# A linear-attention, gated and routed kernel: the first loads in another order, and the product of w3 and w_out one step sooner

## The chip, the cores and the metric

The kernel runs on one core of one Trainium2 chip. The metric is the device time of one execution in microseconds. Before the change three executions took 2084.07, 2080.27 and 2076.05 us, a median of 2080.27 us.

## What is computed

Three stages follow each other, all in float32.

```
for t in range(S):                      # S = 768, for 4 batches x 8 heads of size 48
    y[t] = r[t] @ (state + outer(u * k[t], v[t]))
    state = w[t][:, None] * state + outer(k[t], v[t])
x  = y as (3072, 384)
x2 = ((x @ w1) * (x @ w2)) @ w3 @ w_out        # w1, w2: 384 x 1024; w3: 1024 x 1024; w_out: 1024 x 384
P  = exp(x2 @ w_gate - max), then 8 rounds of row and column normalising
out = sum over 8 experts e of P[:, e] * (relu(x2 @ W1[e]) @ W2[e])
```

The kernel multiplies w3 by w_out once, at its start, into W (1024 x 384), and uses W for every token.

## The kernel before, in words

The tokens of the first stage are cut into 12 units of 256 tokens (`U`). A loop over steps s, which every engine goes through in its own program, does eight steps per unit (`NF = 8`): for s = 8u + k, TensorE makes the small products of unit u (k = 0: `diag`; k = 1 to 7: `score(u, k - 1)`, one level of a tree that combines decayed blocks), and between them other work. After each `score`, VectorE scales R and K by the decays (`level`, L1105), ScalarE copies R into Rpad (`pad`, L814), and only then can the next `score` run. For u = 1 and later TensorE also closes the unit before (`turn_keys`, `update`, `make_y`).

Beside this, in the first fifteen steps, the weights are prepared. TensorE turns w3 in 16 half rows (`turn_w3`, L1384; two turns for each of the eight 512 KB blocks that `load_w3` fetches into four buffers, `RAW = 4`); ScalarE copies each turned half to SBUF (`copy_w3T`, L859); TensorE makes 64 small products with w_out (`make_W`, L1395), five in a step (`W_EACH = 5`), each seen as two matmul records of 128x384. ScalarE and VectorE split each finished block of W into a high and a low part (`copy_W`, `split_W`), and, in steps 9 to 14, split the six parts of w1 and w2 (`copy_wab`, L869; `split_wab`, L1160). Which turn and which products fall into which step is set by `turns_in` and `W_steps` (L398, L399) from `W_FROM = 3`: turns from step 2 on, products from step 3 to 15.

The second stage follows the first by `LAG = 16`: the first `go_up` (x times w1 and w2) stands in step 15 behind `score(1, 6)` and that step's `make_W`, and waits until all six parts of w1 and w2 are split (`wab_split`, L1501). The first `go_down` (times W) is in step 16 and waits for all of W. From then on each step has one `go_up` and one `go_down`. The routed stage, the longest, comes after the twelve units.

The loads of this stage are issued by SyncE (SP), in program order on one queue: K and R of unit 0 (after VectorE or GpSimd has cleared the tiles: `k_set`, `r_set`), `left`, then, when the decays `Wt` of unit 0 have landed, w3's first block and w_out (L456 to L458). Then K and R of unit 1, w3's second block, Wt of unit 1 and so on, each behind a `scored` or `w3_turned` count (L459 to L486). ScalarE's queue carries u, the constants and Wt of unit 0 (L899 to L905). GpSimd's queue loads the experts' weights, the first 576 KB at 37.5 us. TensorE waits for the constants before anything else, and for w_out before the first `make_W` (L1398), and it works strictly in program order: what stands behind a waiting product waits too.

Of the kernel before, what the change touches and what calls it, by code (L numbers as in the profile page):

```python
# [9 lines left out]
def build_program(nc, consts, left, rT, kT, wT, v, uT, moe_w1, moe_w2, moe_w3, moe_w_out, w_gate, w12, out):  # L10
# [10 lines left out]
    B, H, HD, S = rT.shape  # L21
# [9 lines left out]
    HROW = 64  # L31
# [10 lines left out]

    LAG = 16
    W_FROM = 3
    SLICES = NF * U
    RAW = 4
    TURNED = 4
# [43 lines left out]
    with ExitStack() as ctx:  # L92
# [4 lines left out]
        def sb(name, shape, dt=f32, at=None):  # L97
            if at is None:
                at = top[0]
                top[0] += size_of(shape)  # L100
            return nc.alloc_sbuf_tensor_at(name, shape, dt, offset=at)

        def sem(name):
            return ctx.enter_context(nc.semaphore(name))
# [18 lines left out]
        const_sb = sb("const_sb", [P, P + SUB + 2])  # L123
        ident = const_sb[:, 0:P]
        ident32 = const_sb[:, P:P + SUB]
        usel_sb = sb("usel_sb", [P, 2, PAIRS])
# [16 lines left out]
        R = [sb(f"R{p}", [P, PAIRS * CT]) for p in range(2)]  # L143
# [31 lines left out]
        def end_of(limit):  # L175
# [71 lines left out]
        k_loaded, r_loaded, v_loaded = ([sem(f"{n}_loaded{p}") for p in range(2)] for n in ("k", "r", "v"))  # L247
        wab_loaded = [sem(f"wab_loaded{m}") for m in range(2)]
        w3_loaded = [sem(f"w3_loaded{i}") for i in range(RAW)]
        w_loaded, u_loaded, consts_loaded, left_loaded, wout_loaded, wg_loaded, first_loaded, p_stored = map(  # L250
            sem, ["w_loaded", "u_loaded", "consts_loaded", "left_loaded", "wout_loaded", "wg_loaded", "first_loaded", "p_stored"])
        p_loaded = [sem(f"p_loaded{i}") for i in range(2)]
        w2_loaded = [sem(f"w2_loaded{i}") for i in range(2)]
        k_set, k1_set, r_set, rp_set, rp_first, rp_begun, warm_set, w_set, u_set, cleared, w3_turned, w3T_copied = map(
            sem, ["k_set", "k1_set", "r_set", "rp_set", "rp_first", "rp_begun", "warm_set", "w_set", "u_set", "cleared", "w3_turned", "w3T_copied"])
        W_made, W_hi_made, W_split, wab_hi_made, wab_split = map(
            sem, ["W_made", "W_hi_made", "W_split", "wab_hi_made", "wab_split"])
        ruk_made, diag_made, near_set, near_done, scored, r_scaled, k_scaled, decayed, rp_copied = map(
            sem, ["ruk_made", "diag_made", "near_set", "near_done", "scored", "r_scaled", "k_scaled", "decayed", "rp_copied"])
# [24 lines left out]
        PAIR_LOAD = 16 * 2  # L284
        pair_no = lambda u: u // 2 + 1
        level_no = lambda u, l: NL * u + l + 1
# [62 lines left out]
        def last_projection(n):  # L349

            v, o = divmod(n, 6)
            st, _, end = SPANS[v]
            f = NF * end - 1
            G = group_of(st, f)
            return 3 * (block_no(G) + 2 * (f - first_f(G))) + o
# [41 lines left out]

        turns_in = lambda s: [i for i in range(2 * NF) if W_FROM - 1 + HB * i // W_EACH == s]  # L398
        W_steps = lambda s: range(W_EACH * max(0, s - W_FROM), max(0, min(W_EACH * (s + 1 - W_FROM), NF * NF)))  # L399
        W_in = lambda s: [f for f in range(NF) if NF * f + NF - 1 in W_steps(s)]  # L400
# [9 lines left out]
        def part(src, u, h):  # L410
            b, n = divmod(u, UB)
            return src[b, h::2, :, CT * n:CT * n + CT].rearrange("g d t -> d g t")

        rows_of = lambda t, h: by_pair(t[HROW * h:HROW * h + HD, :])
# [3 lines left out]
        def _(sp):  # L418
            def load_k(u):
                for h in range(2):  # L420
                    sp.dma_start(rows_of(K[u % 2], h), part(kT, u, h)).then_inc(k_loaded[u % 2], 16)

            def load_r(u):
                for h in range(2):
                    sp.dma_start(rows_of(R[u % 2], h), part(rT, u, h)).then_inc(r_loaded[u % 2], 16)
# [5 lines left out]
            def load_v(u):  # L431
                b, n = divmod(u, UB)
                sp.dma_start(V[u % 2][:, :, :], v[b, CT * n:CT * n + CT, :].rearrange("(c p) d -> p c d", p=P)).then_inc(v_loaded[u % 2], 16)

            def load_w3(f):
                sp.dma_start(w3_raw[f % RAW][:, :], moe_w3[P * f:P * f + P, :]).then_inc(w3_loaded[f % RAW], 16)

            def load_wab(i, w):
                own = w[0:2 * LAST * HD, :].rearrange("(t h e) f -> h e t f", h=2, e=HD)
                gap = w[2 * LAST * HD:D, :].rearrange("(h t q) f -> h q t f", h=2, q=GAP)  # L440
                for h in range(2):
                    sp.dma_start(wab_raw[HROW * h:HROW * h + HD, i, :, :], own[h]).then_inc(wab_loaded[i], 16)
                    sp.dma_start(wab_raw[HROW * h + HD:HROW * h + HROW, i, :, :], gap[h]).then_inc(wab_loaded[i], 16)
# [6 lines left out]

            sp.wait_ge(k_set, 1)
            load_k(0)
            sp.wait_ge(r_set, 1)
            load_r(0)
            sp.dma_start(left_sb[:, :, :], left).then_inc(left_loaded, 16)
            sp.wait_ge(w_loaded, PAIR_LOAD)  # L456
            load_w3(0)
            sp.dma_start(wout_raw[:, :, :], moe_w_out.rearrange("(j p) d -> p j d", p=P)).then_inc(wout_loaded, 16)  # L458
            sp.wait_ge(scored, level_no(0, 0))  # L459
            sp.wait_ge(k1_set, 1)  # L460
            load_k(1)
            sp.wait_ge(r_set, 2)
            load_r(1)
            load_w3(1)
            sp.wait_ge(decayed, level_no(0, 0))
            sp.wait_ge(scored, level_no(0, 1))
            load_w(1)
# [2 lines left out]
            load_v(0)  # L470
            sp.wait_ge(scored, level_no(0, 3))
            load_w3(3)
            sp.wait_ge(scored, level_no(0, 4))
            load_wab(0, moe_w1)
            sp.wait_ge(scored, level_no(0, 5))
            sp.wait_ge(w3_turned, 2)
            load_w3(RAW)
            sp.wait_ge(scored, level_no(0, 6))
            sp.wait_ge(w3_turned, 4)
            load_w3(RAW + 1)  # L480
            load_v(1)
            sp.wait_ge(w3_turned, 6)
            load_w3(RAW + 2)
            load_wab(1, moe_w2)
            sp.wait_ge(w3_turned, 8)
            load_w3(RAW + 3)  # L486
            assert NF == RAW + 4

            for u in range(1, U + 1):
# [320 lines left out]
        def _(act):  # L810
            def copy(dst, src):
                return nc.scalar.activation(dst, src, ACT.Copy)  # L812
# [83 lines left out]

            act.wait_ge(warm_set, 1)
            copy(warm[:, 1:2], warm[:, 0:1])
            act.wait_ge(u_set, 1)  # L899
            for h in range(2):  # L900
                act.dma_start(usel_sb[HROW * h:HROW * h + HD, h, :], uT[h]).then_inc(u_loaded, 16)
            act.dma_start(const_sb[:, :], consts).then_inc(consts_loaded, 16)
            act.wait_ge(w_set, 1)
            for h in range(2):
                act.dma_start(rows_of(Wt, h), part(wT, 0, h)).then_inc(w_loaded, 16)  # L905
# [172 lines left out]
        def _(dve):  # L1078
            ve = nc.vector
# [92 lines left out]

            ve.memset(warm[:, 0:1], 0.0).then_inc(warm_set, 1)
            ve.memset(K[0][:, :], 0.0).then_inc(k_set, 1)
            ve.memset(Wt[:, :], 0.0).then_inc(w_set, 1)
            ve.memset(usel_sb[:, :, :], 0.0).then_inc(u_set, 1)

            def split_xs(st, p):
                what = x_tile(st, X_OWN[p]) if p in X_OWN else xw[:, :] if p == S3 else xs_sum[:, p, :]
# [568 lines left out]
```

## Time and profile before

| what | value |
|---|---|
| median of three executions | 2080.27 us |
| the profiled execution, its own time | 2073.27 us |
| its span in the trace | 2071.4 us |
| TensorE busy | 2012.6 us, 97% |
| VectorE, ScalarE, GpSimd busy | 66%, 38%, 30% |
| mean DMA traffic | 153 GB/s |

All times below are microseconds from the start of the span. A line of the timeline has start, duration, engine, source line, operation, the tiles written and read, shape, and in brackets how long the engine had been idle and what it waited for. SPq and ACTq lines are issues of DMAs. Matmul ends are modelled.

### The profile page before, as it was taken

What the parts mean: (1) busy time and instruction counts of PE and PEld (TensorE: products, weight loads), DVE (VectorE), ACT (ScalarE), POOL (GpSimd) and SP (SyncE); (2) the same over time, 40 slices, a digit from 0 to 9 for tenths busy, and PEclk for the clock granted to TensorE, in tenths of its full rate; (3) what the DMA queues carried; (4) which work ended last, traced back from release to release, by engine and by line L of the source; (5) the groups of instructions that cost most, each with busy time, mean ns of one, the idle gap of its engine ahead of it and who ended that gap; (6) DMA issues with size and microseconds to landing.
All of it is one profiled execution on the core that took longest, in us unless ns stands there. A gap on an engine that the chain in (4) does not pass through costs nothing.

```text
span 2071.4 us, 40274 instructions
## 1 busy us (share of the span) xinstructions
PE 2012.6 (97%) x16048; PEld 1672.6 (81%) x16048; DVE 1357.8 (66%) x2129; ACT 790.9 (38%) x1448; POOL 614.1 (30%) x879
## 2 busy tenths in 40 slices
PE   6899999999999999999989999999999999999999
PEld 4699999999777777787868888888877888888887
DVE  3677777783686777777676556655676665566556
ACT  4555554553433333333433333332333333333332
POOL 2466776760565666762030000000020000000000
PEclk9999999999999999999999999999999999999999
DMA  8443343330366676775433444343443445443442
GB/s 214 108 122 98 114 130 99 109 104 18 101 229 224 222 248 241 250 256 200 170 122 132 171 146 161 122 167 136 155 140 113 150 140 175 138 160 132 152 137 97
DMA packets 118585, 316.11 MB, mean 153 GB/s; under 512 B 11920, under 2 KB 45616, under 8 KB 118400
## 3 DMA queue, kind: packets, MB, share of 16 engines
q1 hardware_dynamic: 102768, 259.38, 38.7%
q0 software_dynamic: 14944, 53.68, 7.5%
q8 instruction: 128, 2.10, 0.4%
q10 hardware_dynamic: 688, 0.48, 0.1%
q14 instruction: 57, 0.47, 0.1%
HBM read 239.87 MB, written 71.27 MB: 150 GB/s over the span
## 4 chain that ended last, share of the span: by engine, by line
PE 84%; DVE 8%; issue 3%; ACT 2%; DMA 1%; SPq 0%; POOL 0%; DVEq 0%; ACTq 0%
PE ps L1576 22%; PE ps L1578 22%; PE ps L1577 21%; PE ps L1380 4%; PE ps L1381 3%; PE ps L1382 3%; PE ps L1453 2%; PE ps L1403 2%; DVE tb L1306 1%; DVE xs_lo L1082 1%; PE ps L1492 1%; PE ps L1494 1%; DVE tb L1269 1%; DVE R L1117 1%; ACT h_hi L1009 1%
## 5 line engine op out<-in xcount | busy, mean ns | idle before, releaser
L1009 ACT ACTIVATE h_hi<-tb 128x512 fp32r<-128x512 f32 x378 | 239.0, 632 | 651.4 <-DVE tb L1306 619.8
L1576 PE MATMUL ps<-h_hi,w 128*128 128x512 f32 x1152 | 454.7, 395 | 4.2 <-DVE h_lo L1274 4.0
L1578 PE MATMUL ps<-h_hi,w 128*128 128x512 f32 x1152 | 455.3, 395 | 0.0
L1577 PE MATMUL ps<-h_lo,w 128*128 128x512 f32 x1152 | 454.0, 394 | 0.0
L812 ACT ACTIVATE tb<-ps 128x512 f32<-128x512 f32 x378 | 224.8, 595 | 332.2 <-PE ps L1578 325.9
L1274 DVE SCALAR_TENSOR_TENSOR h_lo<-tb,h_hi 128x512 fp32r<-128x512 f32 x382 | 281.3, 736 | 98.6 <-ACT h_hi L1009 79.6
L1265 DVE TENSOR_TENSOR tb<-tb,ps 128x512 f32<-128x512 f32 x252 | 172.1, 683 | 227.7 <-PE ps L1578 227.3
L1269 DVE TENSOR_TENSOR tb<-ps,tb 128x512 f32<-128x512 f32 x252 | 172.8, 686 | 148.1 <-PE ps L1578 148.1
L1306 DVE SCALAR_TENSOR_TENSOR tb<-tb,Pb 128x512 f32<-128x512 f32 x348 | 253.8, 729 | 18.1
L1576 PEld LDWEIGHTS ps<-h_hi,w 128*128 128x128 f32 x1152 | 216.2, 188 | 57.6 <-issue 7.6
L1577 PEld LDWEIGHTS ps<-h_lo,w 128*128 128x128 f32 x1152 | 217.3, 189 | 50.6
L1578 PEld LDWEIGHTS ps<-h_hi,w 128*128 128x128 f32 x1152 | 216.2, 188 | 49.5
L1576 PE MATMUL ps<-xs_hi,early 128*128 128x512 f32 x504 | 201.3, 399 | 5.7 <-DVE tb L1265 3.0
L738 POOL TENSOR_TENSOR xs_sum<-x 128x512 f32<-128x512 f32 x21 | 34.6, 1660 | 559.3 <-PE ps L1578 559.1
L1578 PE MATMUL ps<-xs_hi,early 128*128 128x512 f32 x504 | 200.0, 397 | 0.0
L1577 PE MATMUL ps<-xs_lo,early 128*128 128x512 f32 x504 | 198.4, 394 | 0.0
L1576 PE MATMUL ps<-xs_hi,late 128*128 128x512 f32 x441 | 174.5, 396 | 8.8 <-DVE tb L1269 5.8
L1578 PE MATMUL ps<-xs_hi,late 128*128 128x512 f32 x441 | 173.2, 393 | 0.0
L1577 PE MATMUL ps<-xs_lo,late 128*128 128x512 f32 x441 | 172.8, 392 | 0.0
L812 ACT ACTIVATE Rpad<-R 64x512 f32<-64x512 f32 (+1 forms) x170 | 110.6, 650 | 162.4 <-DVE R L1117 155.1
L1380 PE MATMUL ps<-x,wab_hi 128*128 128x256 f32 x576 | 171.0, 297 | 1.0 <-DMA x<-yT 1.0
L1382 PE MATMUL ps<-x,wab_lo 128*128 128x256 f32 x576 | 161.8, 281 | 0.0
(159 smaller groups left out, 3299.7 us busy)
## 6 DMA issues: line engine op xcount, KB each, us to landing
early<-w_rows SPq DMA_DIRECT2D x63, 1024.0 KB, 5.5
late<-w_rows SPq DMA_DIRECT2D x63, 896.0 KB, 5.2
w<-w_rows SPq DMA_DIRECT2D x128, 384.0 KB, 4.3
w_rows<-batch POOLq DMA_DIRECT2D x105, 384.0 KB, 3.6
w_rows<-w SPq DMA_DIRECT2D x64, 384.0 KB, 2.7
Pb<-p_rows SPq DMA_DIRECT2D x24, 512.0 KB, 6.0
w_raw<-w POOLq DMA_DIRECT2D x16, 576.0 KB, 6.0
w_raw<-w SPq DMA_DIRECT2D x16, 576.0 KB, 4.7
```

What stands on the lines that cost most here:

```text
L812: return nc.scalar.activation(dst, src, ACT.Copy)
L1009: nc.scalar.activation(h_hi[:, slot_of(G, b), :], tb[:, t_of(G, b), :], ACT.Relu).then_inc(h_hi_made, 1)
L1265: ve.tensor_tensor(t, t, bank, ALU.subtract).then_inc(added, 1)
L1269: ve.tensor_tensor(t, bank, t, ALU.add).then_inc(added, 1)
L1274: ve.scalar_tensor_tensor(out=h_lo[:, slot, :], in0=what, scalar=0.0, in1=h_hi[:, slot, :].bitcast(f32), op0=ALU.max, op1=ALU.subtract).th ...
L1306: ve.scalar_tensor_tensor(out=t, in0=what, scalar=0.0, in1=Pb[k % 2][:, 1 - b % 2, :], op0=ALU.max, op1=ALU.mult).then_inc(scaled, 1)
L1380: mm(o, w_hi, x_hi, start=start, stop=False, skip_group_check=shared)
L1381: mm(o, w_hi, x_lo, start=False, stop=False, skip_group_check=shared)
L1382: return mm(o, w_lo, x_hi, start=False, stop=stop, skip_group_check=shared)
L1576: mm(o, w_hi, x_hi, start=start, stop=False, skip_group_check=True)
L1577: mm(o, w_hi, x_lo, start=False, stop=False, skip_group_check=True)
L1578: return mm(o, w_lo, x_hi, start=False, stop=stop, skip_group_check=True)
```

## The change

SP first loads K, then u, the constants and `left`, and, waiting for nothing more, w3's first block and w_out. R of unit 0 moves to ScalarE's queue, ahead of Wt; VectorE clears `usel_sb` before `Wt`. w3's second block goes ahead of K and R of unit 1. The gates' weights (`load_wab`) move behind w3's fifth and sixth blocks (the w1 half) and behind its last (the w2 half), and the waits for `scored(0, 4)` and `scored(0, 6)` go. `W_FROM = 2` moves every turn of w3 and every product of W one step sooner: turns in steps 1 to 13, products in steps 2 to 14.

```
-    W_FROM = 3
+    W_FROM = 2
@@ SP
             load_k(0)
-            sp.wait_ge(r_set, 1)
-            load_r(0)
+            sp.wait_ge(u_set, 1)
+            for h in range(2):
+                sp.dma_start(usel_sb[HROW * h:HROW * h + HD, h, :], uT[h]).then_inc(u_loaded, 16)
+            sp.dma_start(const_sb[:, :], consts).then_inc(consts_loaded, 16)
             sp.dma_start(left_sb[:, :, :], left).then_inc(left_loaded, 16)
-            sp.wait_ge(w_loaded, PAIR_LOAD)
             load_w3(0)
             sp.dma_start(wout_raw[:, :, :], moe_w_out.rearrange("(j p) d -> p j d", p=P)).then_inc(wout_loaded, 16)
             sp.wait_ge(scored, level_no(0, 0))
+            load_w3(1)
             sp.wait_ge(k1_set, 1)
             load_k(1)
             sp.wait_ge(r_set, 2)
             load_r(1)
-            load_w3(1)
...
             load_w3(3)
-            sp.wait_ge(scored, level_no(0, 4))
-            load_wab(0, moe_w1)
             sp.wait_ge(scored, level_no(0, 5))
             sp.wait_ge(w3_turned, 2)
             load_w3(RAW)
-            sp.wait_ge(scored, level_no(0, 6))
             sp.wait_ge(w3_turned, 4)
             load_w3(RAW + 1)
+            load_wab(0, moe_w1)
             load_v(1)
             sp.wait_ge(w3_turned, 6)
             load_w3(RAW + 2)
-            load_wab(1, moe_w2)
             sp.wait_ge(w3_turned, 8)
             load_w3(RAW + 3)
+            load_wab(1, moe_w2)
@@ ScalarE
-            act.wait_ge(u_set, 1)
+            act.wait_ge(r_set, 1)
             for h in range(2):
-                act.dma_start(usel_sb[HROW * h:HROW * h + HD, h, :], uT[h]).then_inc(u_loaded, 16)
-            act.dma_start(const_sb[:, :], consts).then_inc(consts_loaded, 16)
+                act.dma_start(rows_of(R[0], h), part(rT, 0, h)).then_inc(r_loaded[0], 16)
             act.wait_ge(w_set, 1)
@@ VectorE
             ve.memset(K[0][:, :], 0.0).then_inc(k_set, 1)
+            ve.memset(usel_sb[:, :, :], 0.0).then_inc(u_set, 1)
             ve.memset(Wt[:, :], 0.0).then_inc(w_set, 1)
-            ve.memset(usel_sb[:, :, :], 0.0).then_inc(u_set, 1)
```

## Rows read from the trace of the kernel before

**Rows 1.** The page: engines' busy time, and shares of the chain that ended last.
```profile
PE 2012.6 (97%) x16048; PEld 1672.6 (81%) x16048; DVE 1357.8 (66%) x2129; ACT 790.9 (38%) x1448; POOL 614.1 (30%) x879
...
PE 84%; DVE 8%; issue 3%; ACT 2%; DMA 1%; SPq 0%; POOL 0%; DVEq 0%; ACTq 0%
```

**Rows 2.** Stretches: PE, PEld, DVE, ACT, POOL busy; granted clock; DMA share; GB/s.
```profile
0.00:26.44 26.44, 9.59 (x274) 7.20 (x274) 11.03 (x20) 8.63 (x12) 10.24 (x12) 1.00 0.87 204
26.44:62.44 36.00, 36.00 (x578) 24.48 (x579) 16.45 (x31) 20.02 (x36) 4.22 (x6) 1.00 0.94 202
62.44:64.86 2.42, 0.00 (x0) 0.00 (x0) 1.00 (x1) 1.36 (x2) 0.00 (x0) 1.00 1.07 237
64.86:92.00 27.14, 24.27 (x357) 16.57 (x356) 19.16 (x29) 14.99 (x24) 11.87 (x13) 1.00 0.27 68
...
98.00:640.00 542.00, 530.46 (x8667) 486.75 (x8666) 387.74 (x681) 263.99 (x547) 331.41 (x496) 1.00 0.39 117
```

**Rows 3.** Timeline of TensorE and VectorE from 8 to 28 us.
```profile
8.50 1.29 DVE L1094 TENSOR_TENSOR ruk<-K,R 128x512 f32<-128x512 f32 x2 [5.46 <-DMA R<-rT]
...
10.77 1.08 PE L1453 MATMUL ps<-Rpad,K 128*32 128x32 f32 x64
...
14.14 1.09 PE L1453 MATMUL ps<-Rpad,K 128*32 128x32 f32 x64 [2.29 <-ACT Rpad L812]
15.24 1.97 PE L1392 MATMUL ps<-const_sb,w_raw 128*128 128x128 f32 x8
...
17.48 1.08 PE L1453 MATMUL ps<-Rpad,K 128*32 128x32 f32 x64 [0.28 <-issue]
...
20.34 3.49 PE L1403 MATMUL ps<-wout_raw,w3T 128*128 128x384 f32 x10 [1.77 <-DMA wout_raw<-moe_w_out]
...
26.44 0.66 PE L1392 MATMUL ps<-const_sb,w_raw 128*128 128x128 f32 x4 [2.61 <-DMA w_raw<-moe_w]
...
27.03 0.77 PE L1453 MATMUL ps<-Rpad,K 128*32 128x32 f32 x64
...
40.16 1.04 PE L1392 MATMUL ps<-const_sb,w_raw 128*128 128x128 f32 x8
```

**Rows 4.** DMA issues at 3.4, 4.9, 11.3, 27.8 and 52.8 us: KB, us to landing.
```profile
R<-rT SPq DMA_DIRECT2D x1, 192.0 KB, 5.0
...
Wt<-wT ACTq DMA_DIRECT2D x1, 192.0 KB, 6.0
...
wout_raw<-moe_w_out SPq DMA_DIRECT2D x1, 1536.0 KB, 9.0
...
w_raw<-moe_w SPq DMA_DIRECT2D x1, 512.0 KB, 4.0
...
R<-rT SPq DMA_DIRECT2D x2, 192.0 KB, 15.2
```

**Rows 5.** Stretches by DMA traffic, columns as in Rows 2.
```profile
11.90:18.20 6.30, 3.77 (x125) 3.30 (x129) 4.63 (x8) 3.49 (x6) 0.00 (x0) 1.00 1.02 350
...
33.30:53.20 19.90, 19.90 (x278) 13.42 (x277) 7.08 (x15) 11.14 (x22) 3.75 (x5) 1.00 1.03 235
```

**Rows 6.** Timeline of 72 to 92 us: the end of the preparation of the weights.
```profile
72.13 0.68 DVE L1094 TENSOR_TENSOR ruk<-K,R 128x512 f32<-128x512 f32 x1
...
76.58 0.60 ACT L812 ACTIVATE w3T<-ps 128x512 f32<-128x512 f32 x1 [0.51 <-PE ps L1392]
...
87.21 1.27 ACT L812 ACTIVATE Rpad<-R 64x512 f32<-64x512 f32 x2 [3.22 <-DVE R L1117]
...
88.50 0.49 ACT L812 ACTIVATE W_hi<-ps 128x384 fp32r<-128x384 f32 x1
...
89.60 2.85 PE L1403 MATMUL ps<-wout_raw,w3T 128*128 128x384 f32 x8
...
90.59 1.25 DVE L1082 TENSOR_TENSOR wab_lo<-wab_raw,wab_hi 128x1024 fp32r<-128x1024 f32 x1 [1.01 <-ACT wab_hi L812]
...
91.99 0.57 PE L1380 MATMUL ps<-x,wab_hi 128*128 128x256 f32 x1
```

More of the change, by code:

```diff
@@ L44, in build_program @@
     LAG = 16
-    W_FROM = 3
+    W_FROM = 2
     SLICES = NF * U
@@ L452, in _ @@
             load_k(0)
-            sp.wait_ge(r_set, 1)
-            load_r(0)
+            sp.wait_ge(u_set, 1)
+            for h in range(2):
+                sp.dma_start(usel_sb[HROW * h:HROW * h + HD, h, :], uT[h]).then_inc(u_loaded, 16)
+            sp.dma_start(const_sb[:, :], consts).then_inc(consts_loaded, 16)
             sp.dma_start(left_sb[:, :, :], left).then_inc(left_loaded, 16)
-            sp.wait_ge(w_loaded, PAIR_LOAD)
             load_w3(0)
@@ L459, in _ @@
             sp.wait_ge(scored, level_no(0, 0))
+            load_w3(1)
             sp.wait_ge(k1_set, 1)
@@ L463, in _ @@
             load_r(1)
-            load_w3(1)
             sp.wait_ge(decayed, level_no(0, 0))
@@ L472, in _ @@
             load_w3(3)
-            sp.wait_ge(scored, level_no(0, 4))
-            load_wab(0, moe_w1)
             sp.wait_ge(scored, level_no(0, 5))
@@ L477, in _ @@
             load_w3(RAW)
-            sp.wait_ge(scored, level_no(0, 6))
             sp.wait_ge(w3_turned, 4)
             load_w3(RAW + 1)
+            load_wab(0, moe_w1)
             load_v(1)
@@ L483, in _ @@
             load_w3(RAW + 2)
-            load_wab(1, moe_w2)
             sp.wait_ge(w3_turned, 8)
             load_w3(RAW + 3)
+            load_wab(1, moe_w2)
             assert NF == RAW + 4
@@ L898, in _ @@
             copy(warm[:, 1:2], warm[:, 0:1])
-            act.wait_ge(u_set, 1)
+            act.wait_ge(r_set, 1)
             for h in range(2):
-                act.dma_start(usel_sb[HROW * h:HROW * h + HD, h, :], uT[h]).then_inc(u_loaded, 16)
-            act.dma_start(const_sb[:, :], consts).then_inc(consts_loaded, 16)
+                act.dma_start(rows_of(R[0], h), part(rT, 0, h)).then_inc(r_loaded[0], 16)
             act.wait_ge(w_set, 1)
@@ L1174, in _ @@
             ve.memset(K[0][:, :], 0.0).then_inc(k_set, 1)
+            ve.memset(usel_sb[:, :, :], 0.0).then_inc(u_set, 1)
             ve.memset(Wt[:, :], 0.0).then_inc(w_set, 1)
-            ve.memset(usel_sb[:, :, :], 0.0).then_inc(u_set, 1)
             def split_xs(st, p):
```

## The prediction

> **What bounds the kernel now.** I read the page first. TensorE is busy 97% of the span and carries 84% of the chain that ended last [rows 1], so an edit counts only by how much sooner TensorE gets through its program. The stretches say where it is not full: 9.59 of the first 26.44 us, everything from there to 62.44, nothing in 2.42 us at 62.44, 24.27 of 27.14 up to 92.00, then 530.46 of 542 [rows 2]. The change touches only what lies ahead of 92 us; behind that TensorE runs with 98% busy on the same instructions, so a shift of the first `go_up` (91.99) passes to the end one for one. The timeline of the head [rows 3] gives its waits: ruk from 8.50 (R landed), the second score at 14.14, the first `make_W` at 20.34 (w_out landed), the second turn at 26.44 (w3's second block landed).
>
> The whole head idle is 16.85 us, and of what the edits can reach (26.44 - 8.50) only a few us can go. 0.5% of the time, about what a measurement of this kernel can tell from no change, is 10.4 us. That settles most of the chances.
>
> **R on ScalarE's queue, constants behind K.** Before, K and R stand on one queue, u, constants and Wt on the other. R's second half is issued at 3.38 and lands 5.0 later, at 8.4; the last of Wt, from 4.9, + 6.0 = 10.9 [rows 4]. All of it is 1152 + 121 = 1273 KB in the 7 us from the first data (about 3.9) to 10.9: 182 GB/s, and the bytes are the same after the change. What changes is the order. K and R, 768 KB, now come first with nothing between: 768 / 182 = 4.2 us, so 8.1 at this rate; since K was already moving before R's first issue, and some 0.15 MB of the other queue no longer goes ahead, I take 7.5. Constants and `left` follow at about 8.5 to 9.3 (they landed at 9.1 before), so ruk runs at 7.5 to 8.8 and the first score about 1 us sooner, from 9.8 instead of 10.77. Bounds: 0 to 1.2 us sooner.
>
> **Wt behind R, beside w3.** Wt shares the DMA engines with constants and then with w3, whose rows are 4 KB against 1 KB. Alone it would land at 10.5; with w3's 512 KB ahead of it entirely, 512 / 350 = 1.5 us later [rows 5], 12.0. I take 11.5. The first decay scaling began at 11.91, so the head gains 0.4 there (from +0.1 to -1.1), and the second score moves to about 13.8. Little hangs on it: behind it comes the wait for w_out [rows 3].
>
> The Trainium skill (DMA: Bandwidth & Descriptors, "Issuing engines are not separate DMA queues") states that transfers started by different engines interleave on the same 16 DMA engines, and that a second issuing engine saves only issue time. The two queues' 182 GB/s together agree. By that rule alone R would gain 0.7 us (its earlier issue), by mine 0.9, and neither reaches TensorE's end.
>
> **w3's first block and w_out.** This is the term that counts. They were issued at 10.91 and 11.30; data moved from 11.90 to about 18.2 at 350 GB/s [rows 5], and w_out landed at 11.3 + 9.0 = 20.3 [rows 4]: 6.3 us of transfer and 2.1 of tail. Now they stand behind the rest with no pause: the engines are through with the first 1273 KB at about 10.6 instead of idling to 11.9. So w_out lands at 10.6 + 6.3 + 2.1 = 19.0, 1.3 us sooner, though it is issued 6 us sooner: the transfer, not the issue, was the limit. Bounds: 17.0 (the first loads mix with the long rows and nothing of the tail stays) to 20.3.
>
> **One step sooner.** Turns 0 and 1 now stand behind the first score. w3's block lands at 12.5 to 13, the turns take 1.97 [rows 3] and end by 15, which can push the second score to 15; it is still ahead of w_out. But the third score, which ran at 17.48 while TensorE waited for w_out, now stands behind the first `make_W` and waits with it. From w_out's landing to the score of step 4 TensorE now has: five products 3.42 (steady advance; the row shows 3.49), turn 0.53, score 0.69, five products 3.42, turn 0.45, some 8.5 in all, so the score of step 4 begins at 19.0 + 8.5 = 27.5; before it began at 27.03. TensorE is thus 0.5 later by the step, and one block of products ahead. w3's second block, now directly behind w_out, lands 1.5 to 2 us after it, before the turn needs it at 22.4, so the wait of 2.61 is gone: it has been filled by nothing new, the 5 products that stood behind it are now those that came before.
>
> Steps 4 to 14 have the same score work and number of turns as before (ten up to step 11), so the 0.5 stays until step 12. What is saved is the work left out at the end: step 14 has four products instead of five (0.68) and step 15 none of its four, 2.78 (eight records [rows 6]). If TensorE were the bound there, `go_up` would start 0.5 - 0.7 - 2.8 = -3.0 us later, that is 3.0 sooner.
>
> **Why most of it does not arrive.** `go_up` also waits for the sixth split part of w1 and w2. The row of that split ends at 90.59 + 1.25 = 91.84, 0.15 ahead of `go_up` [rows 6]: both waits end together. That chain runs ScalarE, VectorE, ScalarE through steps 12 to 14: w3T copy at 76.58 (which waits for TensorE's turn in step 12, and still does), wab part, scaling, Rpad copy at 87.21, W_hi 0.40, w3T 0.60, wab part 1.06, VectorE's part. One step sooner takes the w3T copy out of step 14 (-0.6), keeps W_hi (block 7 for block 6), and puts W_hi in front of the part of step 13 (+0.4), where nothing hides it. Sum -0.2 to -0.3. TensorE's own work ends at about 90.1, and it then waits 1.5 us for the split. So `go_up` starts at 91.99 - 0.3 + 0.5 = 92.2.
>
> **The gates' weights behind w3.** w1's half was issued from 32.4, now at about 38 (with SP's wait for `scored(0, 5)`); from 31.8 (27.8 + 4.0 [rows 4], w3's fourth block) to 38 the queue then lies idle, where from 33.3 on 4.7 to 4.9 us of transfer took place. The bytes up to w3's seventh block are the same and ran from 33.3 to 53.2 without a pause [rows 5], so that block lands at about 58.1; it is needed at about 61 (step 10). w1's half, two transfers earlier, lands at some 55, and its first part is copied at 56.7. w2's half, last in line now, lands near 70 and is needed at 77.2, behind the w3T copy [rows 6]. R of unit 2 landed at 52.83 + 15.2 = 68.0 [rows 4]; 72.9 now, needed by VectorE at 72.13 [rows 6]: 0.3 us late even with everything 0.5 later, and hidden, as the score that follows had 0.9 to spare. All covers are thin (1.7 to 3 us); without them each late us costs one. I take 0, bounds 0 and +3.
>
> **Sum.** w_out and the third score +0.5, ScalarE's copies -0.3, queue 0: +0.2 us. The profiled execution would take 2073.3 + 0.2 = 2073.5 us; the median of the three is 7.0 above that execution, so I put 0.2 on the median: 2080.5 us.
>
> **Rivals.**
>
> A. The products run at the lower clock: slower. The granted clock is shown as 1.00 (2.4 GHz) all along [rows 2], but until 18.6 TensorE's instructions take longer: eight turns 1.97 us against 1.04 later, a score 1.08 against 0.77 [rows 3], about the 1.2 GHz level. At 20.34 the products are fast. Before that TensorE had been busy for 4.1 of the 4.4 us from 14.14 to 18.56. Now the third score is gone from there, and TensorE idles from about 15 to 19.0 just before the block. If the block runs slow, by the turns' ratio of 1.9 it costs 3.1 us (half of it: 1.5). It decides if the clock is low at w_out's landing. `go_up` +1.7 to +3.3, time 2082 to 2084. Against it: the idle 2.6 us before 26.44 cost no clock. The Trainium skill (TensorE: Matmul & The Clock Gate, Part 1) states that the low clock is the default and comes back with idleness, which speaks for this rival; the trace's slow early rows agree with the default.
>
> B. The head is really 3 us or more shorter. w_out at 17 (-2.0), and the 2.42 us hole at 62.44, in which TensorE waited for none of its inputs while the DMA engines were full (share 1.07, [rows 2]), does not come back, as the traffic lies otherwise (-2.4). But R of unit 2 at 72.9 and the split of w1 and w2 hold the front back; of 4.4 some 2 to 3 would arrive: 2077.5 to 2078.5. For it: the hole stands in saturated traffic.
>
> C. The thin covers tear: R of unit 2 or w3's seventh block late by 3 us, or a second hole as at 62.44. Slower by 2.4 to 5: 2083 to 2085.5. For it: 4.9 us of transfer time given away; against: every need I could date is still met.
>
> **Numbers.** Forecast (within 1 us of no change) 0.42; A 0.25; B 0.18; C 0.15. All lie within 0.5% of the median, so the chances follow from what none of them holds: faster by over 0.5% 0.02, slower 0.03, within 0.95. The cases span 2077.5 to 2085.5; the three executions before span 8 us, so a median of three can sit 4 us off. Range 2073 to 2088.
>
> **What would show it.** In the trace after: w_out lands between 18.4 and 19.6; the first 128x384 product starts there, with the third score behind it; the score of step 4 begins at 27.5 (30 or later if A holds, with products over 3.6 us per ten); no wait for w3's second block; no 128x384 product behind the score of step 15, and in its place 1 to 2 us of TensorE idle that ends with VectorE's last wab_lo; R of unit 2 lands at 72 to 74. The forecast is wrong if `go_up` starts before 90.5 or after 93.5, or if the time behind 98 us changes by more than 2 us.

## The result: 0.27% slower, and the profile after

| | before | changed |
|---|---|---|
| median of nine executions | 2076.99 us | 2082.72 us |
| lowest, highest | 2072.16, 2084.07 | 2081.32, 2086.62 |
| the profiled execution, its span | 2073.27, 2071.4 us | 2081.45, 2079.6 us |

The ratio is 1.0027, 95% interval 1.0014 to 1.0040: some 5.7 us slower, under the 0.5% that was set as the bound of no change, but clear of noise (the interval is 2.9 to 8.3 us). The forecast was 2080.5 us, a change of +0.2.

First the stretches of the changed kernel (columns as in [rows 2]: TensorE, weight loads, VectorE, ScalarE, GpSimd busy; granted clock; DMA share; GB/s).

```profile
0.00:26.44 26.44, 12.40 (x284) 9.04 (x285) 10.32 (x19) 9.05 (x13) 9.07 (x11) 0.94 0.98 218
26.44:62.44 36.00, 36.00 (x550) 24.30 (x549) 16.75 (x32) 19.33 (x36) 5.19 (x7) 1.00 0.71 181
62.44:92.00 29.56, 23.79 (x360) 15.59 (x358) 17.34 (x27) 13.01 (x19) 7.28 (x8) 0.88 0.38 82
92.00:98.00 6.00, 2.33 (x21) 2.09 (x22) 5.38 (x7) 4.31 (x9) 5.47 (x8) 0.88 0.18 66
98.00:200.00 102.00, 100.86 (x2014) 95.59 (x2013) 74.14 (x129) 53.62 (x109) 70.80 (x111) 0.99 0.40 120
```

Up to 62.44 TensorE does a little more than before; behind it, until 98, 26.12 of 35.56 us are busy where 30.27 were. The granted clock, 1.00 everywhere in [rows 2], reads 0.94 in the first stretch and 0.88 there (part of each stretch at 1.2 GHz). Behind the head nothing that can be told apart changes: from 120 to 2000 us TensorE is busy 1848.5 us in one and 1848.2 in the other. The two spans differ by 8.2 us, 6.1 of them up to the score of step 17 (99.36 before, 105.41 now). The remaining 2.1 lie within the scatter of the traces: from that score to the end it takes 1972.0 to 1976.6 us in the fourteen traces of this document, in no order of the kernels.

The timeline of TensorE shows where it goes; these lines answer [rows 3] and [rows 6].

```profile
11.20 1.03 PE L1413 MATMUL ps<-usel_sb,ruk 128*32 128x2 f32 x64 [11.20 <-DMA const_sb<-consts]
...
15.47 0.76 PE L1451 MATMUL ps<-Rpad,K 128*32 128x32 f32 x64 [0.56 <-issue]
...
18.51 4.95 PE L1401 MATMUL ps<-wout_raw,w3T 128*128 128x384 f32 x10 [2.28 <-DMA wout_raw<-moe_w_out]
...
23.83 0.76 PE L1451 MATMUL ps<-Rpad,K 128*32 128x32 f32 x64
...
28.38 0.76 PE L1451 MATMUL ps<-Rpad,K 128*32 128x32 f32 x64
...
63.34 0.32 PE L1451 MATMUL ps<-Rpad,K 128*32 128x32 f32 x13
...
67.20 0.96 PE L1451 MATMUL ps<-Rpad,K 128*32 128x32 f32 x51 [3.54 <-issue]
...
68.09 5.75 PE L1401 MATMUL ps<-wout_raw,w3T 128*128 128x384 f32 x10
...
87.44 0.77 PE L1445 MATMUL ps<-Rpad,K 128*32 128x32 f32 x64 [1.29 <-DVE K L1117]
...
94.01 1.09 PE L1451 MATMUL ps<-Rpad,K 128*64 128x128 f32 x16 [2.77 <-DVE K L1117]
...
96.77 0.58 PE L1378 MATMUL ps<-x,wab_hi 128*128 128x256 f32 x1 [1.66 <-DVE wab_lo L1080]
...
100.52 0.71 PE L1413 MATMUL ps<-usel_sb,ruk 128*32 128x2 f32 x64
```

Read against the rows of before: the first product starts at 11.20 and not at 9.90; w_out has landed at 18.5 and not at 20.3, but ten records then take 4.95 us instead of 3.49; the score of step 4 stands at 28.38 (27.03). The pause inside step 11's score, 2.43 us before, is 3.54, and the block behind it takes 5.75 us. Ahead of the first `go_up` there are now 2.77 and 1.66 us of idle time, and from its start to the next diag it takes 3.75 us instead of 2.49 (91.99 to 94.48).

Last, landings that answer [rows 4]: the constants, w_out, and half of R of unit 2, issued at 3.9, 5.3 and 54.2.

```profile
const_sb<-consts SPq DMA_DIRECT2D x1, 81.0 KB, 7.3
...
wout_raw<-moe_w_out SPq DMA_DIRECT2D x1, 1536.0 KB, 13.2
...
R<-rT SPq DMA_DIRECT2D x1, 192.0 KB, 18.5
```

### The profile page after: what moved, and what is told of

It reads as the page before. It is cut to its first block, busy times and chain, and to the rows that moved or that the text cites. A ratio compares the mean times of both kernels' runs of the same rounds, so it can differ in the third digit from the quotient of the medians.

```text
span 2079.6 us, 40272 instructions
## 1 busy us (share of the span) xinstructions
PE 2019.8 (97%) x16048; PEld 1676.6 (81%) x16048; DVE 1361.0 (65%) x2129; ACT 791.0 (38%) x1448; POOL 610.7 (29%) x879
## 4 chain that ended last, share of the span: by engine, by line
PE 83%; DVE 9%; issue 4%; ACT 3%; DMA 1%; SPq 0%; POOL 0%; DVEq 0%; ACTq 0%
PE ps L1574 21%; PE ps L1576 21%; PE ps L1575 21%; PE ps L1378 4%; PE ps L1379 3%; PE ps L1380 3%; PE ps L1451 2%; PE ps L1401 2%; DVE tb L1304 2%; PE ps L1490 1%; DVE xs_lo L1080 1%; DVE tb L1267 1%; ACT h_hi L1007 1%; PE ps L1492 1%; DVE h_lo L1272 1%
## 5 line engine op out<-in xcount | busy, mean ns | idle before, releaser
L1272 DVE SCALAR_TENSOR_TENSOR h_lo<-tb,h_hi 128x512 fp32r<-128x512 f32 x382 | 282.1, 739 | 98.7 <-ACT h_hi L1007 79.6
L1378 PE MATMUL ps<-x,wab_hi 128*128 128x256 f32 x576 | 171.6, 298 | 2.9 <-DVE wab_lo L1080 1.7
L1379 PE MATMUL ps<-x,wab_hi 128*128 128x256 f32 x576 | 162.4, 282 | 0.0
```

The source lines that it names most:

```text
L1272: ve.scalar_tensor_tensor(out=h_lo[:, slot, :], in0=what, scalar=0.0, in1=h_hi[:, slot, :].bitcast(f32), op0=ALU.max, op1=ALU.subtract).th ...
L1378: mm(o, w_hi, x_hi, start=start, stop=False, skip_group_check=shared)
L1379: mm(o, w_hi, x_lo, start=False, stop=False, skip_group_check=shared)
```

## The experiments

All were timed in five rounds beside the kernel before. Milestones of each trace, in us: start of the first matmul; start of the first block of products of w3 and w_out / its length (3.49 at the high clock); score of step 4; the pause inside step 11's score, at one fixed place of TensorE's program (below); first `go_up`; first score of unit 2 (step 17), which closes what is called the head here.

| kernel | ratio, 95% interval | start | first block | step 4 | pause | go_up | step 17 |
|---|---|---|---|---|---|---|---|
| before | | 9.9 | 20.3 / 3.5 | 27.0 | 2.4 | 92.0 | 99.4 |
| before again | 1.0005 (0.9996-1.0015) | 9.6 | 20.3 / 6.3 | 27.0 | 2.7 | 92.3 | 99.7 |
| changed | 1.0027 (1.0014-1.0040) | 11.2 | 18.5 / 5.0 | 28.4 | 3.5 | 96.8 | 105.4 |
| changed again | 1.0031 (1.0020-1.0043) | 11.0 | 16.5 / 5.8 | 27.2 | 2.7 | 94.3 | 105.3 |
| e1 products back | 1.0005 (0.9995-1.0015) | 11.0 | 19.4 / 3.5 | 23.2 | 5.4 | 97.2 | 104.5 |
| e2 products only | 1.0058 (1.0046-1.0070) | 10.2 | 20.1 / 5.5 | 30.5 | 2.7 | 103.4 | 114.8 |
| e3 gates early | 1.0033 (1.0021-1.0045) | 10.9 | 16.5 / 5.4 | 26.8 | 1.9 | 97.1 | 108.0 |
| e4 first loads back | 1.0022 (1.0013-1.0031) | 11.0 | 16.3 / 4.1 | 25.3 | 3.1 | 93.7 | 104.9 |
| e5 fill tail | 1.0014 (1.0005-1.0022) | 10.8 | 16.3 / 3.5 | 25.4 | 1.7 | 96.6 | 104.0 |
| e6 fill both | 1.0022 (1.0013-1.0031) | 11.0 | 17.1 / 3.4 | 25.4 | 2.4 | 97.7 | 105.0 |
| e7 less traffic | 1.0003 (0.9992-1.0013) | 9.9 | 20.6 / 5.2 | 27.1 | 1.3 | 91.4 | 98.7 |
| e8 changed, less traffic | 1.0031 (1.0021-1.0042) | 11.1 | 16.6 / 3.5 | 25.1 | 6.2 | 97.5 | 108.7 |
| e9 gates between | 1.0012 (1.0000-1.0024) | 11.2 | 20.0 / 3.8 | 24.1 | 0.4 | 95.7 | 103.1 |
| e10 candidate | 1.0016 (1.0006-1.0026) | 11.1 | 19.7 / 3.5 | 23.6 | 2.4 | 96.1 | 103.4 |

One trace stands for each kernel, and a pause is one throw (see below); the ratios rest on 5 to 12 executions each.

The last two columns hold the clearest reading of the table, from `go_up` to step 17. Where `W_FROM` is 3 (before, before again, e1, e7, e9, e10) it takes 7.2 to 7.4 us in all six traces. Where it is 2 and nothing fills the emptied places (changed, changed again, e2, e3, e4, e8) it takes 8.6, 11.0, 11.4, 11.0, 11.2 and 11.2. With the places filled (e5, e6) it takes 7.4 again.

### e1: the products back in their steps

```
-    W_FROM = 2
+    W_FROM = 3
```

> All load changes kept, W_FROM back at 3. Theory T1 (the step sooner is what costs: the third score waits behind the first products, TensorE's first block runs at the low clock, and steps 14 and 15 are left with holes that cost the clock again): the third score runs before w_out lands at 18.5, the score of step 4 begins near 23 instead of 28.4, no idle before go_up in step 15; the first go_up starts at 88 to 92 and the kernel is 0 to 4 us faster than before, 5 to 9 us faster than the changed kernel. Rival T2 (the moved gates' weights and the late second hole cost it, whatever W_FROM): go_up at 95 or later, time as changed, +4 to +7 over before.

Measured: 1.0005, nothing that can be told from before, and 2.2 thousandths (4.6 us) under the changed kernel. The third score ran ahead of the products, step 4 came at 23.2, and `go_up` stood directly behind the last products, with no idle time and 7.4 us to the score of step 17, as before. Of T1 the early step 4, the missing idle time and the step as the costly part hold; its sizes do not. It had the kernel 0 to 4 us faster than before and `go_up` at 88 to 92, and `go_up` came at 97.2. T2 had `go_up` right, but its time (as changed) falls. The head was 5 us longer than forecast in this trace, through pauses of 1.45, 1.63 and 5.38 us and a slow block (5.72) behind the last; that execution took 2080.98, 2.2 above the median of its own kernel.

```profile
61.75 0.45 PE L1451 MATMUL ps<-Rpad,K 128*32 128x32 f32 x28
...
67.58 0.75 PE L1451 MATMUL ps<-Rpad,K 128*32 128x32 f32 x36 [5.38 <-issue]
```

### e2: only the products one step sooner

The kernel before with `W_FROM = 2` and nothing else.

> Loads as before, only W_FROM = 2. T1: w_out lands at 20.3, the third score waits for it, the score of step 4 begins at 29 to 30.5 (27.03 before), idle of 1.5 us or more ahead of go_up, which starts at 94 to 97; +3 to +8 us over before. T2: the products' place costs nothing beyond 1 us (both waits of go_up coincide), time within 1 us of before.

Measured: 1.0058, 12 us slower, more than the whole change and more than either theory said. What came on top is in the timeline: the turn of w3's fifth block, one step sooner, waits for that block behind the gates' weights, and the block of products behind that wait runs slow (5.43).

```profile
52.39 1.11 PE L1392 MATMUL ps<-const_sb,w_raw 128*128 128x128 f32 x4 [3.27 <-DMA w_raw<-moe_w]
53.43 1.03 PE L1415 MATMUL ps<-usel_sb,ruk 128*32 128x2 f32 x64
54.40 5.43 PE L1403 MATMUL ps<-wout_raw,w3T 128*128 128x384 f32 x10
```

### e3: the gates' weights where they were

```
+            sp.wait_ge(scored, level_no(0, 4))
+            load_wab(0, moe_w1)
             sp.wait_ge(scored, level_no(0, 5))
             sp.wait_ge(w3_turned, 2)
             load_w3(RAW)
+            sp.wait_ge(scored, level_no(0, 6))
             sp.wait_ge(w3_turned, 4)
             load_w3(RAW + 1)
-            load_wab(0, moe_w1)
...
             load_w3(RAW + 2)
+            load_wab(1, moe_w2)
             sp.wait_ge(w3_turned, 8)
             load_w3(RAW + 3)
-            load_wab(1, moe_w2)
```

> The changed kernel with the gates' weights loaded where they were before. T1: the pause in TensorE at its 852nd matmul record stays (2 to 4 us, at 62 to 67), time within 2 us of the changed kernel. T2: R of unit 2 lands at 68 to 70 instead of 72.6, the pause falls to 2.4 or less and the clock does not drop behind it: 3 to 5 us faster than the changed kernel.

Measured: 1.0033, as the changed kernel. The pause was shorter (1.94), as T2 had it, and the block behind it fast; but the turn of the fifth block waited 2.96 us, as in e2. So moving the gates' weights is not what costs: with the products one step sooner it takes that wait away. With e1, T2 is out.

### e4: the first loads on their queues of before

```
@@ SP
-            sp.wait_ge(u_set, 1)
-            for h in range(2):
-                sp.dma_start(usel_sb[HROW * h:HROW * h + HD, h, :], uT[h]).then_inc(u_loaded, 16)
-            sp.dma_start(const_sb[:, :], consts).then_inc(consts_loaded, 16)
+            sp.wait_ge(r_set, 1)
+            load_r(0)
             sp.dma_start(left_sb[:, :, :], left).then_inc(left_loaded, 16)
             load_w3(0)
@@ ScalarE
-            act.wait_ge(r_set, 1)
-            for h in range(2):
-                act.dma_start(rows_of(R[0], h), part(rT, 0, h)).then_inc(r_loaded[0], 16)
+            act.wait_ge(u_set, 1)
+            for h in range(2):
+                act.dma_start(usel_sb[HROW * h:HROW * h + HD, h, :], uT[h]).then_inc(u_loaded, 16)
+            act.dma_start(const_sb[:, :], consts).then_inc(consts_loaded, 16)
```

> The changed kernel with K, R, left on SyncE's queue and u, constants, Wt on ScalarE's, as before; w3 and w_out still wait for nothing. If the constants behind K and beside R are what made the first product of TensorE late (11.20 against 9.90), it starts at 9.9 to 10.2 here; w_out lands at 18 to 19 as in the changed kernel, and since w_out's landing sets the next wait, the time stays within 1 us of the changed kernel. Rival: the 1.3 us of the start pass through, 1 to 1.5 us faster than the changed kernel.

Measured: 1.0022, not told from the changed kernel, and the start stayed at 11.0, now for R and not for the constants. So the order on the queues is not what made the start late, and the forecast of this run failed. In e10 w3 and w_out are held until R has landed and it is late all the same: Wt is issued at 3.4 instead of 4.5 there, and R's second half, issued at 3.4 as before, lands 6.2 us later instead of 5.0. What is common to all late starts is that Wt is asked for a microsecond sooner, while K, R or the constants are still under way, and that it takes a share of the DMA engines from them fits. It is not shown: no run moved Wt alone, and in e4 and e10 u and the constants are sooner too.

### e5: the emptied places filled

```
+                if s in (14, 15):
+                    fill(3 if s == 14 else 4)      # products into an empty PSUM bank, used by nothing
                 if 0 <= n + 1 < SLICES:
                     go_up(n + 1)
```

> The changed kernel with seven products more that nothing uses (three in step 14 and four ahead of the first go_up in step 15, into an empty PSUM bank), in the place of the products that moved away. Theory: go_up still starts where VectorE's last split lets it (9.3 us behind step 14's score, as in the changed kernel), but TensorE no longer idles 2.8 and 1.7 us just before, so its clock stays high and go_up start to the next diag takes 2.5 us instead of 3.75 to 4.1; 1.5 to 4 us faster than the changed kernel, for more work. Rival: the idle time costs nothing, the added products 0 to 1.5 us slower than the changed kernel.

Measured: 1.0014 against 1.0027 and 1.0031 for the changed kernel, 2.7 to 3.5 us less for 4.8 us more work of TensorE. The intervals overlap (1.0005 to 1.0022 against 1.0014 to 1.0040 and 1.0020 to 1.0043), so the gain in time is likely and not certain. `go_up` started 10.0 us behind step 14's score (9.3 in the changed kernel), so the added products cost their places a little; and from `go_up` to the score of step 17 it took 7.40 us instead of 8.6 and 11.0. The rows of the stretches carry this verdict. From 98 to 106 us the changed kernel ran at 0.69 of the clock in its second trace (0.88 in its first), the filled one at 1.00, the kernel before at 1.00. The lines are, in this order, those of the changed kernel's second trace, of e5 and of the kernel before.

```profile
98.00:106.00 8.00, 8.00 (x166) 7.59 (x165) 2.79 (x5) 3.65 (x8) 7.04 (x15) 0.69 0.22 76
```

```profile
98.00:106.00 8.00, 8.00 (x184) 7.68 (x183) 4.35 (x8) 4.42 (x10) 7.34 (x16) 1.00 0.50 146
```

```profile
98.00:106.00 8.00, 8.00 (x205) 7.46 (x204) 6.89 (x11) 3.56 (x7) 7.18 (x13) 1.00 0.65 183
```

The head was still 4 to 5 us longer than before. TensorE came to step 4 at 25.4, 3 us sooner than in the first trace of the changed kernel, and now the late loads were what it met: a turn waited 1.23 us for w3's seventh block (landed 62.4), and R of unit 2 landed at 76.3, so that VectorE waited 3.81 us for it and TensorE 2.17 us in step 13.

```profile
62.48 0.66 PE L1390 MATMUL ps<-const_sb,w_raw 128*128 128x128 f32 x4 [1.23 <-DMA w_raw<-moe_w]
...
76.41 1.56 DVE L1092 TENSOR_TENSOR ruk<-K,R 128x512 f32<-128x512 f32 x1 [3.81 <-DMA R<-rT]
...
80.82 0.75 PE L1451 MATMUL ps<-Rpad,K 128*32 128x32 f32 x64 [2.17 <-DVE K L1117]
```

### e6: the wait for w_out filled too

```
+                if s == 2:
+                    for i in range(10):
+                        nc.tensor.transpose(ps[:, 3, 0:P], ident, ident)
                 for m in W_steps(s):
                     make_W(m)
```

> As the last, and ten transposes that nothing uses in step 2, while TensorE waits for w_out. Theory: the first block of products takes 3.5 us instead of 4.1 to 5.5, as in the kernels with W_FROM = 3; 1 to 2 us faster than the run with the filled tail. Rival: the transposes push the block back by as much as they save, no difference.

Measured: 1.0022, not faster than e5 (1.0014), and not told by its time from the changed kernel or from e4 (1.0022), where nothing is filled; from `go_up` to step 17 it took 7.4, as in e5. The first block was fast (3.4), but so it was in e5 (3.5), where nothing stood ahead of it; whether that block runs slow differs from trace to trace of one kernel (3.49 and 6.34 before). The rival holds. The run showed something else: with ten more records of TensorE, the pause in step 11's score came ten records of that score sooner (behind 3 instead of 13). Another pause, of 3.21 us, stood in a block of products at 56.4.

### e7 and e8: less traffic ahead of the pause

```
@@ GpSimd
-                if u == FROM_UNIT - 1:
-                    load_w1(0)
...
                 if u + 1 < U:
                     begin_rpad(u + 1)
+                if u == FROM_UNIT - 1:
+                    load_w1(0)
@@ SP
-                    load_w(u + 1)
+                    if u > 1:
+                        load_w(u + 1)
                     sp.wait_ge(y_made, 2 * u)
+                    if u == 1:
+                        load_w(u + 1)
```

> The kernel before with two loads later: the experts' first 576 KB (GpSimd) behind the second Rpad copy, and Wt of unit 2 behind the y of unit 1, 0.96 MB out of the full stretch from 37 to 70 us. 
> The changed kernel with the same two loads later. Theory: pause under 2.5 us instead of 3.5, so the clock does not drop behind it and the following block takes 3.5 instead of 5.75 us: 2 to 4 us faster than the changed kernel. Rival: within 1 us of the changed kernel.

Measured: on the kernel before the pause fell to 1.34 us and `go_up` came at 91.4, but the time did not change (1.0003). On the changed kernel the pause was 6.21 us, the longest of all, and the time 1.0031, as the changed kernel. With 0.96 MB less in the queues the pause can be the shortest and the longest, so the amount of traffic alone does not set it. The theory is not borne out. (Of these lengths each is from one trace.)

```profile
62.28 0.32 PE L1454 MATMUL ps<-Rpad,K 128*32 128x32 f32 x13
68.81 0.96 PE L1454 MATMUL ps<-Rpad,K 128*32 128x32 f32 x51 [6.21 <-issue]
```

### e9 and e10: towards a version that is faster

e9: the changed kernel with `W_FROM = 3`, w3's fifth block and then w1's half at the fifth score, w2's half between w3's seventh and eighth. e10: as e9, with the first loads as in e4, `sp.wait_ge(r_loaded[0], PAIR_LOAD)` ahead of w3's first block, and the two loads of e7 later.

> All load changes but the gates' weights: W_FROM = 3, w3's fifth block first and then the w1 half at the fifth score, the w2 half behind w3's seventh block. Theory: pauses at the 852nd record are longer where the gates' weights (slow, 110 to 180 GB/s) are in flight at 60 to 68 us (3.5, 5.4, 6.2 us against 1.3 to 2.7); here they have mostly passed, the pause is under 2.7 us, the first go_up starts at 90 to 93, time 1 to 4 us under before. Rival: the pause's length is by chance, 3 us or more here too, time +1 as in the run with the products back.

> As the last, with the first loads on their queues of before, w3's first block and w_out held until R has landed, and the experts' first load and Wt of unit 2 later. Theory: TensorE starts at 9.9 instead of 11.0, w_out lands near 18, the pause is under 2 us, go_up at 87 to 90: 2 to 5 us faster than before. Rival: each head start is lost at the next wait (third block of w3, split of the gates' weights): within 1 us of before.

Measured: 1.0012 and 1.0016, both slower than before. Step 4 came 2.9 and 3.5 us sooner, and nothing of it was left at `go_up`. In e9 the pause at the fixed place was 0.40 us, but another of 2.44 us stood 9 us ahead of it, inside `update`, with a block of 5.68 us behind, and one of 1.62 at 45.9. In e10 there were four pauses and two slow blocks (5.18 each). No version here beats the kernel before.

```profile
27.64 1.56 PE L1404 MATMUL ps<-wout_raw,w3T 128*128 128x384 f32 x4 [1.20 <-issue]
...
45.94 0.29 PE L1416 MATMUL ps<-usel_sb,ruk 128*32 128x2 f32 x10 [1.32 <-issue]
...
58.39 0.67 PE L1476 MATMUL ps<-V,Ktok 128*64 128x48 f32 x16 [0.59 <-issue]
...
66.81 0.51 PE L1454 MATMUL ps<-Rpad,K 128*32 128x32 f32 x36 [2.38 <-issue]
```

These places are no accident. Counted in matmul records from the start of the program, they lie behind record 348, 600, 726 and 852: steps of 126, or twice that. It is the same in every trace. Between 20 and 100 us TensorE idles 0.28 us or more with nothing to wait for 31 times in the fourteen traces, and 30 of these lie behind record 348, 600, 726, 852 or 977 (851 for 852 where `W_FROM` is 2; a trace can lack a record). Behind record 852 the pause is always there. At the other places it is there only in the seven traces that came to step 4 at 25.4 or sooner; together the pauses are 8.5 us in e1, 5.5 in e10, 4.8 in e9 and 2.4 in the kernel before. With the slow blocks behind them this is where most of the won time goes.

### e11 and e12: both kernels once more

> The changed kernel once more, on the chip of these runs, for the spread of the pause and of the time. Theory: 4.5 to 7 us over before; start at 11, first block over 4 us, idle 2.8 and 1.7 ahead of go_up as in the first trace; the pause anywhere from 2 to 6 us. Rival: the pause repeats 3.5 within 0.3.

> The kernel before once more, for the same spread. Theory: start 9.9, w_out at 20.3, go_up at 91 to 94, the pause 1 to 4 us. Rival: the pause repeats 2.4 within 0.3.

Measured: 1.0031 and 1.0005. The changed kernel's slowness repeats in a later comparison, and the kernel before against itself shows what such a ratio can be when nothing differs. The score of step 17 repeats within 0.3 us for either kernel (105.4, 105.3; 99.4, 99.7), a difference of 6.1 us in one pair and 5.7 in the other, beside 5.7 of the medians, while what lies within does not repeat: w_out's block 3.49 and 6.34, `go_up` of the changed kernel 96.8 and 94.3. The pauses repeat within 0.3 for the kernel before, as the rival had it, and within 0.8 for the changed one.

## Why the prediction was right, and where it was off

The time lay in the range, and within 0.5% was right. The likeliest case, +0.2 us, was not: +5.7 was measured (interval 2.9 to 8.3), beyond all four cases (C, the farthest, ended at +5). By the prediction's own sign its forecast fails too, as `go_up` was to start at 93.5 at the latest and started at 96.8 and 94.3. That 2080.5 and 2082.72 look close is in part luck: the three executions that set the base had a median 3.3 us above that of all nine. By its steps:

- **Start of the head: wrong sign, without effect by itself.** K and R were to land at 7.5 and the first product to start 1 us sooner; R landed at 7.5 (2.1 + 5.4), but K, alone on the other queue, only at 8.7 and the constants behind it at 11.2 (3.9 + 7.3), and the start was 1.3 and 1.4 us later in the two pairs. I had counted the same bytes in another order; Wt, asked for 1.4 us sooner, was under way beside K and the constants, which fits and was not isolated.
- **w_out at 19.0, 1.3 sooner: right in sign, too small.** It landed at 18.5 in the first trace and at 16.5 in the second, below the bound of 17.0; in the other six traces with the same first loads (e1, e3, e5, e6, e8, e9) it landed at 16.3 to 16.8. The gain is mostly 3.5 to 4 us.
- **The third score behind the first products, step 4 at 27.5: right, the number in part by luck** (28.4 and 27.2). From w_out to that score 8.5 us were forecast and 9.9 and 10.7 measured, as the first block ran slow (4.95, 5.76); the earlier w_out made up for it in the second trace. With `W_FROM = 3` and the same loads it comes at 23.2. The missing wait for w3's second block is right too; that wait had covered the slow first block in the kernel before (6.34 us there and step 4 still at 27.0), and the changed kernel no longer has this cover.
- **ScalarE's chain, -0.3, with `go_up` bound by the split: right to a tenth.** From step 14's score to `go_up` it is 9.33 or 9.34 us in both traces of the changed kernel and in e2, e3 and e4, against 9.61 before (82.38 to 91.99), and VectorE's last split ends the wait, as forecast.
- **The idle time ahead of `go_up`, costed at nothing: the step that failed.** The prediction says that TensorE "then waits 1.5 us for the split" and goes on. It waited 1.66 there and 2.77 (1.58 before) ahead of the score before it, and the clock was low behind it: `go_up` to step 17's score took 8.6 and 11.0 us (e2, e3, e4 and e8 11.0 to 11.4) instead of 7.4. That is 1.3 of the 6.1 us in the first pair of traces and 3.6 of the 5.7 in the second. e5 and e6 put work into these places and it went back to 7.4; e1, where the products stand there again, also has 7.4. The prediction had this mechanism as rival A, priced 1.7 to 3.3 us for another place, the first block. It happened there too, but also in the kernel before (6.34 in one of two traces; 5.2 in e7).
- **The pause inside step 11's score, left out of the sum: size not settled.** At step 12's score the changed kernel was 5.1 and 2.0 us behind before, of which 1.35 and 0.15 were there at step 4. Of the rest the longer pause is 1.1 and 0.0 us, and the slow block behind it (5.75, 4.78 for 3.49) 2.3 and 1.3: here too the low clock is the larger part. The pause's length alone does not decide it, as the block was fast behind 2.70 us in the kernel before and slow behind 2.71 in the changed one. The pause stands at one place of TensorE's program: behind 28 records of a score with `W_FROM = 3` (before, e1, e9), behind 13 with 2, behind 3 with ten records more (e6), which is the same number of records from the start each time. With the steps of 126 records (e10) this speaks against a wait for data and for something that comes with a fixed number of instructions. Inside it the instruction queues move single packets; these are the lines of the changed kernel from 64 to 65 us (packets, MB, share of 16 engines).

```profile
q8 instruction: 1, 0.02, 10.3%
q14 instruction: 1, 0.01, 5.9%
```

  That TensorE waits there for its next instructions fits; no run separates it further, and the trace does not say which queue serves TensorE. The Trainium skill (Runtime: NRT & Kernel Launch, "Instruction fetch mechanics") states that each engine refills its instructions in 16 KB blocks over its own DMA queue, mostly hidden. The packet of q8 here is one of 0.02 MB; hidden it was not at this place. But what makes it 0.4, 1.3 or 6.2 us long was not found: less traffic gave both ends. It stays open.
- **The gates' weights: covers held, thinly.** w3's seventh block landed at 61.0 (58.1 forecast) for a turn at 62.8, R of unit 2 at 72.7 (72.9 forecast) and, in the second trace, at 74.5, where VectorE waited 0.16 us for it. Rival C's torn covers did not occur in the changed kernel, as its TensorE was late itself; in e5, where it was sooner, both tore. What the prediction missed is that this move is needed: without it (e2, e3) the fifth block's turn waits 3 us, as it stands one step sooner.

The parts do not add in time: the products alone +12 us, all loads with the products back +1, together +5.7. The product's step is the part that costs, 4.6 us in company of the loads.

The Trainium skill (TensorE: Matmul & The Clock Gate, Part 1) states that idleness brings the low clock back; the rows agree here: granted clock 0.69 and 0.88 (second and first trace) behind the two idle times, 1.00 with the places filled.

## What to carry to other kernels

Work that is taken out from in front of a wait leaves idle time, and on TensorE this is not free: ask whether the clock will be high behind it, at the place where the wait ends, and not only where the new wait begins. When a part of a schedule is moved one step sooner, look for whatever waited behind its old first wait (here a score that used to run free), and for the loads that it now needs a step sooner. A load that is issued sooner may be paid for by those beside it. And a head start counts only where the next wait, or the next pause, does not take it back.

## What the runs showed of the hardware that was not expected

- Filler work can keep the clock up: with seven unused products ahead of `go_up`, which put it 0.7 us later, the stretch behind took 7.4 us instead of 8.6 to 11.4. The whole kernel was 2.7 to 3.5 us faster by its ratio in e5, with overlapping intervals, and 1.0 to 1.9 in e6.
- A pause of 0.4 to 6.2 us at a fixed count of TensorE's matmuls, with no wait of the program at that place, in all fourteen traces, and others of 0.3 to 3.2 us at 126 records or a multiple from it in seven of them.
- The first block of products took 3.49 and 6.34 us in two traces of one kernel: the clock that TensorE is granted at one place of the program differs from execution to execution.
